# Moving one small tile from in front of four scratch tiles to behind them, in an attention + two-mixture kernel

## The reference

```
attn:   q_s = softmax over the 64 features;  k_s = softmax over the 576 positions
        kv = k_s^T v (64 x 64 per head);  out = q_s kv         4 batches, 8 heads
moe:    a = x w1;  b = x w2;  h = (a * b) w3;  x = h w_out     x is 2304 x 512, d_ff 1024
moe2:   p = domain_probs / (sum + 1e-9)                        4 experts
        out = sum over e of p[:, e] * (relu(x w1[e]) w2[e])    w1[e] 512 x 1024, w2[e] 1024 x 512
```

## Time and profile before

| | |
|---|---|
| median of three runs | 1201.16 us |
| the profiled execution | 1201.16 us, of which its instructions span 1199.3 us |
| PE busy | 1164.0 us, 97% of the span, 6112 matmuls |
| DVE, ACT, POOL busy | 611.0, 295.5, 298.4 us |
| PE's mean granted clock | 0.988 of full speed |
| HBM read and written | 41.46 and 4.72 MB |

### The profile page before, as it was taken

One profiled execution on the slowest core, in us unless ns is written; L12 is line 12 of the kernel. 1 busy time (PEld: TensorE's weight loads), 2 busy tenths in 40 slices (PEclk: granted clock), 3 DMA queues, 4 the chain that ended last, 5 costly groups with the idle time before them and its releaser, 6 DMA issues.

```text
span 1199.3 us, 15947 instructions
## 1 busy us (share of the span) xinstructions
PE 1164.0 (97%) x6112; PEld 1070.0 (89%) x6112; DVE 611.0 (51%) x900; ACT 295.5 (25%) x565; POOL 298.4 (25%) x358
## 2 busy tenths in 40 slices
PE   7788999999999989999999999999999999999998
PEld 5676899999999988899999999999999999999997
DVE  5987432121221395555555555555555555555555
ACT  4435531121211233222212111122222222212111
POOL 2334610000000311422322323323223223224210
PEclk9898899999999999999999999999999999999999
DMA  9695320000000100100101001000001001010012
GB/s 271 138 176 125 83 71 1 1 0 0 0 0 0 36 0 1 36 18 18 35 0 35 18 17 35 17 17 35 17 17 35 17 18 35 0 35 25 11 53 105
DMA packets 45453, 46.56 MB, mean 39 GB/s; under 512 B 22640, under 2 KB 36976, under 8 KB 45424
## 3 DMA queue, kind: packets, MB, share of 16 engines
q1 hardware_dynamic: 45424, 46.18, 14.1%
HBM read 41.46 MB, written 4.72 MB: 38 GB/s over the span
## 4 chain that ended last, share of the span: by engine, by line
PE 89%; DVE 5%; DMA 3%; ACT 2%; issue 1%; SPq 0%; DVEq 0%
PE b_ring L1071 8%; PE b_ring L1072 8%; PE b_ring L1070 8%; PE b_w L1070 7%; PE b_w L1072 7%; PE b_w L1071 7%; PE b_kv L1072 5%; PE b_kv L1071 5%; PE b_kv L1070 5%; PE b_w3t L1070 4%; PE b_w3t L1071 4%; PE b_w3t L1072 4%; PE b_kmax L1070 4%; PE b_kmax L1072 4%; PE b_kmax L1071 4%; DMA kb<-in_k 2%
## 5 line engine op out<-in xcount | busy, mean ns | idle before, releaser
L1031 DVE SCALAR_TENSOR_TENSOR acc<-b_ring,pg,acc 128x512 f32<-128x512 f32 x180 | 135.1, 751 | 109.1 <-PE b_ring L1072 109.1
L412 POOL TENSOR_SCALAR uf<-stage 128x256 fp32r<-128x256 f32 x48 | 19.6, 408 | 564.6 <-PE b_kmax L1072 232.6
L1071 PE MATMUL b_ring<-u,hT 128*128 128x512 f32 x384 | 149.7, 390 | 0.0
L1072 PE MATMUL b_ring<-u,hT 128*128 128x512 f32 x384 | 149.6, 389 | 0.0
L1070 PE MATMUL b_ring<-u,hT 128*128 128x512 f32 x384 | 149.4, 389 | 0.0
L615 ACT ACTIVATE hT<-b_w 128x384 fp32r<-128x384 f32 x72 | 35.4, 492 | 449.4 <-DVE b_w L1009 445.2
L1031 DVE SCALAR_TENSOR_TENSOR acc<-b_kv,pg,acc 128x512 f32<-128x512 f32 x90 | 67.6, 751 | 60.4 <-PE b_kv L1072 60.3
L1071 PEld LDWEIGHTS b_ring<-u,hT 128*128 128x128 f32 x384 | 72.1, 188 | 15.6
L1070 PEld LDWEIGHTS b_ring<-u,hT 128*128 128x128 f32 x384 | 72.1, 188 | 15.4
L1072 PEld LDWEIGHTS b_ring<-u,hT 128*128 128x128 f32 x384 | 72.1, 188 | 15.1
L1072 PE MATMUL b_kv<-u,hT 128*128 128x512 f32 x192 | 75.5, 393 | 0.0
(11 more groups left out here) (170 smaller groups left out, 2773.9 us busy)
## 6 DMA issues: line engine op xcount, KB each, us to landing
stage<-in_moe_w SPq DMA_DIRECT2D x40, 512.0 KB, 3.3
qb<-in_q SPq DMA_DIRECT2D x4, 1152.0 KB, 9.7
kb<-in_k SPq DMA_DIRECT2D x4, 1152.0 KB, 9.7
vb<-in_v SPq DMA_DIRECT2D x32, 144.0 KB, 3.8
out<-acc SPq DMA_DIRECT2D x18, 256.0 KB, 2.0
stage<-in_moe_w SPq DMA_DIRECT2D x16, 256.0 KB, 3.3
wraw<-in_moe_w_out SPq DMA_DIRECT2D x4, 512.0 KB, 6.8
pr<-in_moe_domain_probs SPq DMA_DIRECT2D x1, 36.0 KB, 4.0
```

What stands on the lines that cost most here:

```text
L412: nc.gpsimd.tensor_scalar(uf[:, form, HI], of, 1.0, 0.0, ALU.mult, ALU.add).then_inc(pool_hi, 1)
L1031: nc.vector.scalar_tensor_tensor(acc[:, tile, :], O_BANK[t % TT], scale, acc[:, tile, :], ALU.mult, ALU.add).then_inc(acc_added, 1)
L1071: nc.tensor.matmul(ps, w_hi_, x_lo_, start=False, stop=False, skip_group_check=onto)
L1072: return nc.tensor.matmul(ps, w_lo_, x_hi_, start=False, stop=stop, skip_group_check=onto)
```

## The change

`pg` goes from in front of `u2` to behind `snap`. The other four tiles move down by 640 bytes (576 of `pg` and the 64 unused), and keep their order.

```
     EX = SM + 1408
-    pg = at("pg", [P, NT, NG // 2], F32, EX)
-    U2 = EX + 640
-    u2 = at("u2", [P, 2, 2, DM], F32R, U2)
-    sums = at("sums", [P, 4, 2, P], F32, U2 + 8192)
-    snap = at("snap", [P, 3, TB], F32, U2 + 12288)
-    b11_last = at("b11_last", [P, 2, TB], F32, U2 + 12288)
+    u2 = at("u2", [P, 2, 2, DM], F32R, EX)
+    sums = at("sums", [P, 4, 2, P], F32, EX + 8192)
+    snap = at("snap", [P, 3, TB], F32, EX + 12288)
+    b11_last = at("b11_last", [P, 2, TB], F32, EX + 12288)
+    pg = at("pg", [P, NT, NG // 2], F32, EX + 16896)
```

## The result

| | before | changed |
|---|---|---|
| median of eight runs | 1201.88 us | 1212.26 us |
| the profiled execution, and its span | 1201.16, 1199.3 us | 1208.86, 1207.1 us |
| PE busy | 1164.0 us | 1172.3 us |

The ratio on record is 1.0076, 95% interval 1.0061 to 1.0090: 7 to 11 us slower. (The quotient of the two medians in the table, 1.0086, lies in that interval.) The forecast was 1201.2 us with a range of 1197 to 1206, and had 0.90 on no change. It was wrong.

The account below looks back on a forecast made before the run. PE was taken as the bound, busy 97% of the span. The 1199.3 us span plus 1.9 us around it, plus five terms of 0, gave 1201.2 us, range 1197 to 1206.

Parts of the forecast that it names:

- the term for `u2`: PE's 1728 matmuls reading `u2` in the projections: no longer or shorter at the new address, 0 us.
- the two things that "speak on addresses": Uniform 389 to 395 ns over four `u2` addresses, and nine `wout` matmuls also taking 2.08 us: no address effect.
- the irregularity of the first nine matmuls: Start of each projection: nine matmuls at 231 ns each instead of 227, ascribed to the change of width.
- The bounds: Limits on the `u2` matmuls: +5 us at the first nine's pitch, +22 us at the longest step, -22 us if faster.
- Rival 1: Projection matmuls slower because another engine works at an address sharing something with `u2`; +10 us, 1212 us, chance 0.04.
- Rival 2: ACT's `snap` writes taking twice as long, ending after PE wants the bank; +7 us, 1208 us, chance 0.01.
- the terms for `pg`, `sums`, the writing of `u2` and `b11_last`: DVE's scale reads, POOL's work and DVE's short chain before the first slot: no change, 0 us each.
- Rival 3: `u2`'s old address costs time now: -3 us (1198) or -22 us (1179) saved; chance of the large one 0.02.
- the test the prediction set itself: Forecast wrong if the stretch after 447 us differs by more than 3 us; the matmuls on `u` say which rival.

Follow-up runs that it names:

- e9: Changed kernel with only `hT` (and behind it `stage` and the small tiles) 128 bytes higher, so `u2` minus `hT` is 0 modulo 256; ratio 0.9993 to the kernel before.
- e4: Changed layout with `u2`, `sums`, `snap` and `pg` at its addresses, every other tile moved up by 384 bytes; ratio 0.9982 to the kernel before.
- e13: Changed kernel with only the low half of `u2` 128 bytes off against `hT`, the high half at difference 0; 1209.1 us, 8.40 us a projection.
- e10: Kernel before with only `uf`, stationary operand of the 384-column block products, moved up 128 bytes; ratio 1.0039, 4.7 us.

## Why the prediction was wrong

**The step that failed is the term for `u2`**, "Value taken: 1728 x 0 = 0 us". It measured 48 x 0.198 us = 9.5 us in the projections, less 48 x 0.018 = 0.9 us in the six matmuls behind each, 8.6 us in all. What the term left out is that the pitch of a matmul depends on where its moving tile lies against the weights that PE loads beside it.

**What was wrong in its reasoning** were the two things that "speak on addresses". The four parts of `u2` that showed one duration lie 2048 bytes apart: they are one address as far as 256 bytes go. And `wout`, offered as a tile "over 160,000 bytes away" with the same times, starts at 13,440 and 50,304, both 128 modulo 256; so do `a_sb` (107,648), `hT` (189,568) and the old `u2` (212,096). The new `u2`, at 211,456, is 0. `xy`, `tx` and `uf` of the earlier trace rows start at 128 as well. In short, every matmul that I took for evidence against an address effect had both its operands at the one residue on which the kernel was built. The evidence was uniform because the sample was. Nor does the irregularity of the first nine matmuls come "with the change of width, not with the address": in e9, where `u2` and `hT` agree but both are 128 off `uf`, it is five steps long instead of nine, and in the changed kernel it is not there at all, the long and short steps begin at once.

**The bounds held, the range did not use them.** I priced a slower pitch at +5, +10 and +22 us and then cut the range to the runs' own scatter, because I read the bounds as all but excluded. The prediction's own sentence, that PE has 5.7 us of slack in 752 and "any such nanosecond is paid in full", was the reason to keep them: the measured 8.6 us lies between the +5 and the +22.

**Rival 1** had the right tile, the right instruction and nearly the right size (+10 us, 1212), at a chance of 0.04, but the wrong partner: it blamed another engine. That its 6 ns come near the measured 5.5 (0.198 us / 36) is luck: it read them off the first three matmuls of a projection, a transient that is there when the addresses agree. The longer steps go through all 36 matmuls alike, whatever DVE, ACT and POOL do, and e4 and e9 cure them by moving PE's own stationary operand.
The Trainium skill ("SBUF — State Buffer", section "Who interferes with whom") gives PE two SBUF read ports, one for the moving operand and one for loading weights, and calls them independent. These runs disagree as to time: 8.20 or 8.40 us a projection, by the address of one relative to the other.

**Rival 2** (`snap`) and the terms for `pg`, `sums`, the writing of `u2` and `b11_last` were right: every duration stayed, as the rows above show, and `b11_last`'s write took 947 ns against 944.

**Rival 3** said that a surplus at the old address might go. The opposite holds: the old difference, 0, is the best of the eight residues tried.

Where the extra time went was forecast by the test the prediction set itself: the stretch after 447 us changed by more than 3 us, and the group of `u` said by what.

## What to carry to other kernels

Where PE is the bound, the byte offset of a matmul's moving tile against the tile whose weights are loaded beside it is part of the design. In the float32r matmuls of these runs a difference that is a multiple of 256 bytes was never the slower one; keep to it, and check it after every change of layout, a harmless one above all. Before calling a resource indifferent to something, ask whether the rows at hand vary in it at all; tiles laid out from one base in multiples of 512 all share one residue. The symptom in a profile is matmuls of one shape whose starts lie 1 to 3% further apart, with no new idle time anywhere.

## What the runs showed of the hardware

- PE's matmuls of 512 columns (float32r, weights loaded for each) start every 227 ns at a difference of 0 modulo 256, and every 233 ns in the mean at 32, 96, 128, 192 and 224; at 160 it is 234, at 64 it is 229. At 384 columns a difference of 128 makes 173.3 into 175.9 ns. The residues other than 0 and 128 were tried with `hT` at one address only.
- The loss does not add up over single reads: one third out of step costs as much as all (e13).
- The partner of the stream is the weight load that runs beside it: one step with `uf` loaded at a difference of 128 takes 232 or 233 ns at the end of a projection that otherwise runs at 227 (e9, e10).
- Left open: what the two operands share, and why 64 is nearly harmless while 32 and 96 are not. A stream without any loading beside it was not tried. Whether the 12 to 13 ns that each matmul takes at any width has the same root was not tested. No variant beats the kernel before by more than e4's 0.2%, which stays unexplained.
